# Releasing weight loads later, moving one weight piece, and copying a group's last x first, in a fused attention and feed-forward kernel

## What is computed

```python
# attention: q, k, v are (2, 8, 768, 64); keep = first n_global keys or 0 <= rel < n_local
scores = q @ k.T / 8 - slope[h] * dist          # masked to -1e9 outside keep
a = softmax(scores)                              # denominator + 1e-9
x = (a @ v) transposed to (2, 768, 512)
# layer 1: w_in (512, 1024), conv_w (3, 1024), w_out (1024, 512)
h = relu(x @ w_in)
x2 = (h * sigmoid(conv3(h))) @ w_out
# layer 2: w_in (512, 1024), w_spatial (768, 768), w_out (512, 512)
u, v = halves of relu(x2 @ w_in);  v_n = layer-normalised v
out = (u * (w_spatial @ v_n + b_spatial)) @ w_out
```

## Time and profile before

| What | us |
|---|---|
| median of 3 runs (360.48 to 360.62) | 360.48 |
| the profiled execution's own time | 360.66 |
| its span in the trace | 358.9 |

### The profile page before, as it was taken

How to read it: one execution, slowest core, us unless ns; L and a number is a source line. 1 busy time by engine, 2 the same in 40 slices (tenths; PEclk the granted TensorE clock), 3 DMA queues, 4 the chain that set the end, 5 groups by cost and what they waited for, 6 DMA issues and landing times.

```text
span 358.9 us, 7396 instructions
## 1 busy us (share of the span) xinstructions
PE 352.8 (98%) x2890; PEld 322.4 (90%) x2891; DVE 216.3 (60%) x572; ACT 177.8 (50%) x451; POOL 90.0 (25%) x165
## 2 busy tenths in 40 slices
PE   8999999999999999999999999999999999999996
PEld 4658998998899999999889999998999999998885
DVE  6996898778785797889693942115853444441000
ACT  4987677776676688562464622114652111112112
POOL 4889897445553000000120300003400000000000
PEclk9999999999999999999999999999999999999999
DMA  7962442333314033312000000010340000001222
GB/s 207 398 248 73 121 132 68 128 101 113 112 46 162 2 117 120 117 30 89 0 2 1 2 0 0 2 44 1 119 150 28 0 0 2 0 2 60 106 100 95
DMA packets 12233, 27.77 MB, mean 77 GB/s; under 512 B 1568, under 2 KB 4256, under 8 KB 12192
## 3 DMA queue, kind: packets, MB, share of 16 engines
q1 hardware_dynamic: 11904, 27.10, 22.5%
q10 hardware_dynamic: 288, 0.13, 0.2%
HBM read 24.08 MB, written 3.15 MB: 76 GB/s over the span
## 4 chain that ended last, share of the span: by engine, by line
PE 87%; DVE 5%; POOL 4%; ACT 3%; issue 1%; DVEq 0%; ACTq 0%; POOLq 0%
PE bank L1588 20%; PE bank L1590 20%; PE bank L1589 20%; PE bank L1544 15%; PE bank L1523 4%; PE bank L1499 3%; PE bank L1453 2%; POOL p_sb L635 2%; ACT p_sb L735 2%; DVE p_sb L1073 2%; POOL w_lo L652 1%; PE bank L1555 1%; DVE denom L1082 1%; DVE c_sb L1110 1%; POOL w_hi L647 1%
## 5 line engine op out<-in xcount | busy, mean ns | idle before, releaser
L1544 PE MATMUL bank<-xT,w_hi 128*128 128x384 f32 x256 | 69.6, 345 | 0.1
L635 POOL TENSOR_SCALAR p_sb<-p_sb,denom 128x256 f32<-128x256 f32 (+1 forms) x96 | 47.9, 511 | 35.7 <-DVE denom L1084 35.7
L735 ACT ACTIVATE p_sb<-p_sb,row_min 128x256 f32<-128x256 f32 (+1 forms) x96 | 46.5, 490 | 14.9 <-DVE row_min L1073 14.9
L1544 PEld LDWEIGHTS bank<-xT,w_hi 128*128 128x128 f32 x256 | 45.7, 188 | 0.8 <-issue 0.5
L1544 PE MATMUL bank<-xT,w_lo 128*128 128x384 f32 x128 | 44.1, 344 | 0.0
L1110 DVE SCALAR_TENSOR_TENSOR c_sb<-h_sb,conv_sb,c_sb 128x382 f32<-128x382 f32 (+1 forms) x64 | 42.1, 658 | 2.3
L1588 PE MATMUL bank<-g_hi,w_hi 128*128 128x386 f32 (+1 forms) x128 | 43.3, 338 | 0.0
L1590 PE MATMUL bank<-g_hi,w_lo 128*128 128x386 f32 (+1 forms) x128 | 43.2, 337 | 0.0
L1589 PE MATMUL bank<-g_lo,w_hi 128*128 128x386 f32 (+1 forms) x128 | 43.1, 336 | 0.0
L656 POOL TENSOR_SCALAR rstd<-mean_var 128x1 f32<-128x1 f32 x12 | 4.7, 390 | 129.2 <-DVE mean_var L1138 129.2
L1073 DVE CUSTOM_DVE_ANT_0 p_sb<-bank,table 128x256 f32<-128x256 f32 (+1 forms) x96 | 33.0, 398 | 4.6 <-PE bank L1453 4.6
(11 more groups left out here) (96 smaller groups left out, 786.3 us busy)
## 6 DMA issues: line engine op xcount, KB each, us to landing
stage<-in_weights SPq DMA_DIRECT2D x17, 512.0 KB, 3.3
v_sb<-in_v SPq DMA_DIRECT2D x8, 390.0 KB, 3.8
k_sb<-in_k SPq DMA_DIRECT2D x8, 384.0 KB, 4.1
out_dram<-out_sb SPq DMA_DIRECT2D x11, 256.0 KB, 2.0
q_sb<-in_q SPq DMA_DIRECT2D x13, 192.0 KB, 2.4
v_sb<-in_v SPq DMA_DIRECT2D x6, 260.0 KB, 4.0
k_sb<-in_k SPq DMA_DIRECT2D x5, 256.0 KB, 2.9
stage_late<-in_weights SPq DMA_DIRECT2D x2, 512.0 KB, 11.2
```

Of the source, the lines that this page charges most:

```text
L635: nc.gpsimd.tensor_scalar(probs_h, probs_h, denom[:, u % SLOTS, h:h + 1], 1.0, ALU.mult, ALU.mult).then_inc(scaled, 1)
L735: nc.scalar.activation(p_sb[:, u % SLOTS, h, 0:n], p_sb[:, u % SLOTS, h, 0:n], ACT.Exp, bias=row_min[:, u % SLOTS, h:h + 1], scale=-1.0, a ...
L1544: last = nc.tensor.matmul(h_bank(j)[:, 0:C], w, x, start=r == 0, stop=r == F1_GROUP - 1)
```

## The change

Four edits. The loads of chunks 1 and 2 wait until triple 0, or triples 0 and 1, are weighed. The load of chunk 3 moves behind the loads of queries and keys for triples 6 and 7, and so behind their waits. The last of the eight pieces (index 7) moves in GpSimd's order from behind unit 22 to behind unit 20, where piece 6 already stands. In triples 4, 8 and 12, `round_x` of the triple before moves from behind the first `copy_pt` to the very front on ScalarE, and `rest_of_x` moves on VectorE from behind three `bias_scores` to behind the first.

```diff
-ROUND_AFTER = {6: 1, 13: 1, 14: 1, 16: 1, 17: 1, 19: 1, 20: 1, 22: 1}
-REST_AFTER = {8: 1, 13: 1, 14: 1, 16: 1, 17: 1, 19: 1, 20: 1, 22: 1}
+ROUND_AFTER = {6: 1, 13: 1, 14: 1, 16: 1, 17: 1, 19: 1, 20: 2}
+REST_AFTER = {8: 1, 13: 1, 14: 1, 16: 1, 17: 1, 19: 1, 20: 2}
...
-            for n in range(1, NW1):
+            for n in range(1, NW1 - 1):
+                sp.wait_ge(weighed, TG * n)
                 load_chunk(n)
             load_queries(HP + 2)
             load_queries(HP + 3)
+            load_chunk(NW1 - 1)
...
             for p in range(HP, ALL_TRIPLES):
                 u = TG * p
+                if p % HP == 0:
+                    round_x(p - 1)
                 for tt in range(TG):
                     if p + 1 < ALL_TRIPLES:
                         soften(u + TG + tt)
                     if tt == 2:
                         relu_h(2 * (p - F1_FIRST))
                     copy_pt(u + tt)
-                    if tt == 0:
+                    if tt == 0 and p % HP:
                         round_x(p - 1)
...
                     if p + 1 < ALL_TRIPLES:
                         bias_scores(u + TG + tt)
-                rest_of_x(p - 1)
+                    if tt == 0 and p % HP == 0:
+                        rest_of_x(p - 1)
+                if p % HP:
+                    rest_of_x(p - 1)
```

## The result

| | before | the change |
|---|---|---|
| median of 6 runs, us | 360.63 (360.48 to 360.95) | 362.24 (361.54 to 362.47) |
| ratio, 95% interval | | 1.0040 (1.0027 to 1.0053) |
| the profiled execution, us | 360.66 | 362.13 |
| its span, us | 358.9 | 360.3 |

The ratio is taken over all runs of both kernels, so it can differ a little from the quotient of the two medians. By it the change is slower by 0.4%, about 1.4 us (1.0 to 1.9); the two medians are 1.6 us apart. The forecast was 1.2 us slower, 361.7 us. The median of 362.24 us lies just above the forecast's own range of 361.2 to 362.2; 0.15 us of the distance is that the kernel before, too, came out higher here than in the three runs that the forecast started from (360.63 against 360.48).

The account below looks back on a forecast made before the run. PE (TensorE) was taken to bound the kernel, its delays in triples 4 to 12 reaching the end in full. Terms 0.8 + 0.0 + 0.4 + 0.0 = +1.2 us on 360.48 gave 361.7 us, own range 361.2 to 362.2.

Parts of the forecast that it names:

- Piece 7: Triple 7: moved piece makes PE stand about 1.1 us at unit 21, old 0.50 us loss goes; +0.8 us.
- margin of 0.64: Unit 21: its probabilities are ready at 51.58 us and PE wants them at 52.22, 0.64 us later.
- The upper end: Piece 7 term at +1.5 us: GpSimd's subtractions and VectorE's taps take turns, unit 21 another 0.9 us later.
- The slow first tap: VectorE's first tap of a block, 1.42 us from 49.06, said to end with GpSimd's subtraction of 48.98 to 50.27.
- old 0.50 us in triple 7: Triple 7 took 8.60 us, 0.50 too long; said to go once piece 7 is not before units 22 and 23.
- Triple 4: x copied first: its wait goes, but unit 13's transposes come 0.30 us late; 0.0 us, from -0.3 to +0.2.
- the 0.33 us: Triple 4 took 8.43 us, 0.33 us too long, put down to PE's wait for x.
- Triples 8 and 12: x copied first removes no wait there; PE about 0.1 and 0.3 us late; sum +0.4 us, from 0 to +0.6.
- The loads: Later chunk loads still land in time and relieve early traffic: 0.0 us, from -0.3 to +0.3.
- A: Rival, faster: GpSimd starts unit 18 over 1.1 us sooner and mostly hides piece 7; 359.7 us; chance 0.08.
- B: Rival, no difference: unit 18 starts 0.3 to 0.5 us sooner, triples 8 and 12 cost 0.1; 360.6 us; chance 0.32.
- C: Rival, slower by more: subtractions and taps take turns in full, unit 22's bank late too; 362.6 us; chance 0.15.

Follow-up runs that it names:

- a1_piece: Kernel before with only piece 7 (rounding and subtraction) moved from behind unit 22 to behind unit 20: 361.21 us against 360.62, ratio 1.0018.
- c2_noloads: The change without its later loads: 362.07 us against 360.71 for the kernel before, ratio 1.0036.
- b1_half: Kernel before with only the rounding of piece 7 moved behind unit 20, its subtraction left behind unit 22: 360.42 us against 360.57, ratio 0.9994.
- b2_copyfirst4: Kernel before with ScalarE in triple 4 doing the copy of unit 12, then x, then unit 15's exponentials: 360.73 us against 360.57, ratio 1.0007.
- b4_best: Kernel before with the edits of b2_copyfirst4 and b3_spread together: 361.53 us against 360.57, ratio 1.0022.
- a2_xfirst: Kernel before with only the copy of x and its low part moved to the front in triples 4, 8 and 12: 361.22 us against 360.62, ratio 1.0014.
- a4_xfirst4: Kernel before with the copy of x and its low part moved to the front in triple 4 alone: 360.58 us against 360.62, ratio 1.0000.
- c3_xfirst_all: Kernel before with x copied first in every triple from 4 on: 363.05 us against 360.71, ratio 1.0058.
- a3_loads: Kernel before with only the loads of chunks 1 to 3 released later: 360.85 us against 360.62, ratio 1.0004.
- c4_roundearly: Kernel before with only the roundings of pieces 5, 6 and 7 moved to behind units 17, 19 and 20, subtractions unmoved: 360.61 us against 360.71, ratio 0.9995.
- b3_spread: Kernel before with the last pieces, rounding and subtraction, behind units 17 (two pieces), 19 and 20, none behind 22: 361.17 us against 360.57, ratio 1.0020.

## Why the prediction was right

**Piece 7, +0.8 us forecast: +0.69 in the trace of the change, +0.56 in that of a1_piece.** The same two triples give +0.60 in c2_noloads. The step was GpSimd's extra work of 1.91 us against a margin of 0.64. Counted from triple 4's later start of 0.34, the second head of unit 21 should be ready at 53.83 us at the soonest; it was at 52.71 + 1.23 = 53.94. PE stood 0.89 us in front of unit 21, and the four transposes took 0.90 us in place of 0.66, 1.13 us together for the 1.1 forecast. b1_half bore out the margin. The upper end, GpSimd held up by each tap, did not come: the subtractions took 2.92 us for two, 1.46 each in place of 1.29. It is VectorE that pays more in this pairing (3.06 us for 1.46). Taking turns in full for each overlap, +1.5 us, was too much. The Trainium skill's GPSIMD Engine Reference, section Specifications, says that GpSimd's SBUF interfaces are shared with VectorE; the stretched taps agree with it.

Two readings behind this term were not exact. The slow first tap did not end with the subtraction: it ended at 49.06 + 1.42 = 50.48 us, 0.21 us behind it. And of the old 0.50 us in triple 7, 0.20 us were TensorE's wait for piece 7 itself, which the prediction put down to the order in front of units 22 and 23 alone. Its size and its going were right all the same.

**Triple 4, 0.0 us forecast: 0.00.** Unit 13's transposes came 0.30 us late against unit 12's, as worked out, and the wait for x was gone. What I had not seen is that a third wait stands behind these two: b2_copyfirst4 and b4_best were free of both, and the 0.33 us did not come.

**Triples 8 and 12, +0.4 us forecast: +0.09 and +0.30.** By the medians, a2_xfirst costs 0.5 us and a4_xfirst4 nothing, which gives the same place, and c3_xfirst_all shows the same prices in triples that the change leaves alone.

**The loads, 0.0 us forecast.** a3_loads and c2_noloads leave room for up to some 0.3 us, and show none.

**What was left out: 0.34 us ahead of triple 4.** They are in the trace of the change and nowhere in the sum. The terms that the forecast had come to 0.69 + 0.00 + 0.39 = 1.08 us there, so that its total of 1.2 lies this near to 1.4 is in part luck. Is it an effect of the change? VectorE's sums (`invert_sums`) in the trace before, and in that of the change:

```profile
10.69 0.45 DVE L1082 TENSOR_SCALAR denom<-denom 128x2 f32<-128x2 f32 x1
...
13.71 0.23 DVE L1082 TENSOR_SCALAR denom<-denom 128x2 f32<-128x2 f32 x1
```

```profile
10.64 0.17 DVE L1089 TENSOR_SCALAR denom<-denom 128x2 f32<-128x2 f32 x1
...
13.67 0.50 DVE L1089 TENSOR_SCALAR denom<-denom 128x2 f32<-128x2 f32 x1
```

The same instruction takes 0.17 to 0.50 us, and the two executions part at 10.7 us, ahead of the first instruction that the change moves (the load at 11.96 us before). Triple 4 begins at 28.01 us in c2_noloads and at 28.00 in c4_roundearly, where the loads are as before, and at 27.94 in a3_loads, where they are later; over all fourteen traces it begins between 26.78 and 28.12. So a late start needs no later loads, and this share most likely goes with the execution and not with the edit. It is not shown: all three traces with later loads begin it late (27.89 to 27.94 us), and eight of the eleven others by 27.79. Single runs of the kernel before spread over 360.02 to 361.44 us, which made small gains hard to show.

**The rivals.** A needed GpSimd to start unit 18 1.1 us sooner; it started at 42.03, which is 41.68 before plus the later start of triple 4. B (+0.1 us) lies outside the measured 1.0 to 1.9 us, and none of the earlier starts that it needed came. C's +2.1 us lies outside too; its taking of turns in full did not come.

## What to carry to other kernels

Before work is moved ahead on an engine, read the margin of the first consumer behind the new place, not of the one behind the old place: 0.62 us fitted a margin of 0.64 us, 1.91 us cost more than the two waits (0.5 us) that the move removed. A copy put first so that it is sooner also puts its wait first, and whatever the engine used to do in that wait comes behind it; where a trace shows no wait for the copied data, such a move has only a price. And two engines that slow each other are to be read as a pair: an idle gap on one of them is no free room when the other has work in it that this slows, such as the taps and sums here.

## What was not expected of the hardware

GpSimd's subtraction on 128x512 and VectorE's instructions slow each other unevenly. Beside such subtractions two taps took 2.19 us (one subtraction) or 3.06 us (two) in place of 1.46, and a sum on 128x6 elements 1.25 us, the same shape 0.17 us when free; the subtractions went from 1.29 us only to 1.46 (two in 2.92 us), or 1.57 (two in 3.13). With GpSimd's products it is the other way round. Two rows of the kernel before show a pair of products with no tap beside it, and a pair of taps while GpSimd stood idle:

```profile
52.41 0.93 POOL L635 TENSOR_SCALAR p_sb<-p_sb,denom 128x256 f32<-128x256 f32 x2
...
63.02 1.27 DVE L1110 SCALAR_TENSOR_TENSOR c_sb<-h_sb,conv_sb,c_sb 128x382 f32<-128x382 f32 x2
```

Where the two meet, the products take 1.33 us, 0.40 more, and the taps 1.46, 0.19 more. So the 1.46 us that this document compares with is free of a subtraction, but not of GpSimd.

In the first 28 us, executions of the same code differ in where PE stands by about 1 us: the kernel before and four kernels that edit only the tables behind unit 16 (a1_piece, b1_half, b3_spread, c4_roundearly) begin triple 4 between 26.81 and 28.00 us. The cause of these differences was not found.
